# Decay attention, soft MoE and GELU MLP on one core: the logarithm sums computed on the four quarters of the TensorE array

## The chip, the cores and the metric

The kernel runs on one core of a Trainium2 chip. The metric is the device time of one execution in microseconds (us), as the median of several runs.

## The reference

Three stages follow each other. The change touches the first alone: a linear attention with a decay `w` per token and channel (batch 4, 8 heads, 768 tokens, 48 channels a head).

```python
for t in range(S):
    cur = einsum('bhd,bhe->bhde', u * k_t, v_t)
    y_t = einsum('bhd,bhde->bhe', r_t, state + cur)
    state = w_t[..., None] * state + einsum('bhd,bhe->bhde', k_t, v_t)
x = y as (3072 tokens, 384)
logits = x @ phi; slot_in = softmax_over_tokens(logits).T @ x
slot_out[e] = relu(slot_in[e] @ w1[e]) @ w2[e]
x = softmax_over_slots(logits) @ slot_out
h = x @ w_in; out = (h * sigmoid(1.702 * h)) @ w_out
```

## The kernel before

**Tiling.** The attention is done for 16 pairs of heads. In a pair, head 0 has its 48 channels on partitions 0 to 47 and head 1 on 64 to 111 (`HOFF = 64`, `DP = 112`). The 768 tokens are `NC = 6` chunks of 128. Inside a chunk the recurrence is turned into matmuls: `r` is multiplied by the running product of the decays, `k` by its inverse, both counted from the middle token of the chunk (`MID = 64`). The running products come from sums of logarithms:

- ScalarE takes the logarithm of `w` with tokens on partitions (`logs`, L473, into `lw`).
- TensorE sums them (`log_sum`, L897). One matmul a chunk has `lw` (128 tokens by 112 channels) as weights and streams the constant `tri` (128 by 129). `tri` is -1 for the tokens between `t` and the middle in the early half, 1 for those in the late half, and 0 elsewhere: rows 0 to 63 are zero in columns 65 and up, rows 64 to 127 are zero in columns up to 64, and column 64 is all zero. Three chunks lie in bank 0, three in bank 1.
- ScalarE takes the exponentials (`exps`, L498 into `pinv`, L500 into `pw`), 129 columns a chunk.
- VectorE multiplies (`front`, L701 `k` by `pinv`, L703 `r` by `pw`) and forms the decay of a whole chunk, `fdec` (L705).

An fp32 matmul of the source stands as two MATMUL instructions in the trace.

**Order on TensorE in one pair** (`pair`): transposes of `k` (L977), transposes of `x` for the logits (L917, not in every pair), transposes of the pair before's output (L956), state updates (L992), scores (L1010), in every fourth pair the slot logits (L936), the logarithm sums of the *next* pair (L897), the share of the carried state (L1033, which waits for `scaled`), attention times `v` (L1041).

**Order on ScalarE**: copy of the transposed `k` (L506, L508), copies of transposed `x` (L529), `spread_decay` (L515), `logs` of the next pair (L473, which waits for the load `nat` with `w` in it), `scaled_states` (L523, five activations, for L1033), `exps` of the next pair, and the copies of the output (L570).

**Order on VectorE**: scan over the chunk states (L712), the pair before's output into `x_all` (L749, L751, after which a load may reuse that pair's `nat`), masks (L718), `front` of the next pair, bonus (L735, L738, `av_done`).

**Loads.** All loads go through one queue (SP) in a fixed order. In each pair: `rk` of the pair two ahead (L321, 768 KB, waits until L1033 has run), half of an expert's first weights (L336, 768 KB), in every other pair a piece of `w_early` (L341, 192 KB), `v` and `k` with tokens first (L327, 576 KB, waits for `av_done`), `w` and `r` with tokens first (L332, 576 KB, waits for `x_done`, the end of L751). Both halves of `nat` and `rk` have two buffers.

The soft MoE and the MLP that follow are the same in both kernels. In the first pair everything is done in two halves of three chunks (`first_logs`, `first_log_sums`, `first_exps`, `first_front`).

Of the kernel before, what the change touches and what calls it, by code (L numbers as in the profile page):

```python
# [9 lines left out]
ACT = mybir.ActivationFunctionType  # L10
AX = mybir.AxisListType

P = 128
# [3 lines left out]
def decay_attention_soft_moe_gelu_kernel(nc, rk_in, w0_in, nat_in, u_in, phi_in, w1_in, w2_in, win_in, wout_in, out_t):  # L17
# [9 lines left out]
    NC = S // P  # L27
    PPB = u_in.shape[1]
    B = PAIRS // PPB
    HP = 2  # L30
    HD = u_in.shape[2]
    D = HD // HP
    HOFF = 64
    DP = HOFF + D
# [21 lines left out]
    with top:  # L56
# [3 lines left out]
        def sem(name):  # L60
            return top.enter_context(nc.semaphore(name))
# [97 lines left out]
        const_pool = sem("const_pool")  # L159
        const_dve = sem("const_dve")  # L160
        first_ln = sem("first_ln")
        first_logsums = sem("first_logsums")
# [298 lines left out]
        def _(act):  # L461
# [13 lines left out]

            src = [bank[q][0:DP, 0:G3 * (P + 1)].rearrange("p (c t) -> p c t", c=G3) for q in range(2)]

# [9 lines left out]
            def first_exps():  # L487
                for q in range(2):
                    chunks = slice(G3 * q, G3 * (q + 1))
                    act.wait_ge(logsum_done if q else first_logsums, 1)  # L490
                    a.activation(pinv[0:DP, chunks, :], src[q], ACT.Exp, scale=-1.0).then_inc(inv_done, 1)
                    a.activation(pw[0:DP, chunks, :], src[q], ACT.Exp).then_inc(exp_done, 1)

            def exps(s):
                act.wait_ge(f_done, s.i)
                act.wait_ge(logsum_done, s.i + 1)
                for q in range(2):
                    a.activation(pinv[0:DP, G3 * q:G3 * (q + 1), :], src[q], ACT.Exp, scale=-1.0).then_inc(inv_done, 1)  # L498
                for q in range(2):
                    a.activation(pw[0:DP, G3 * q:G3 * (q + 1), :], src[q], ACT.Exp).then_inc(exp_done, 1)  # L500

# [161 lines left out]
        def _(dve):  # L663
# [6 lines left out]
            v.memset(own[:, :, :], 0.0).then_inc(const_dve, 1)  # L670
            v.memset(frep[:, :], 0.0).then_inc(const_dve, 1)
            v.memset(strip[:, :], 0.0).then_inc(const_dve, 1)
            v.memset(old_peaks, -3.0e38).then_inc(peaks_set, 1)
# [9 lines left out]
            def first_front():  # L683

                dve.wait_ge(ld_rk[0], 16)
                r3, k3 = (rk[0][0:DP, z, :].rearrange("p (c t) -> p c t", c=NC) for z in range(2))
# [196 lines left out]
        def _(pe):  # L883
# [11 lines left out]

            def log_sum(c):
                return t.matmul(bank[c // G3][0:DP, (c % G3) * (P + 1):(c % G3 + 1) * (P + 1)], lw[:, c, 0:DP], tri[:, :],  # L897
                                start=True, stop=True)

            def first_log_sums():  # L900
                for c in range(NC):
                    if c % G3 == 0:
                        pe.wait_ge(ln_done if c else first_ln, 1)
                    ins = log_sum(c)
                    if c == G3 - 1:
                        ins.then_inc(first_logsums, 1)
                ins.then_inc(logsum_done, 1)

            def log_sums(s):
                pe.wait_ge(ln_done, s.i + 1)  # L910
                for c in range(NC):
                    ins = log_sum(c)
                ins.then_inc(logsum_done, 1)
# [49 lines left out]
            def pair(s, b=None, xg=None):  # L963
# [7 lines left out]
                for c in range(NC - 1):  # L971
                    if s.first and c == G3:
                        stay_warm(6, 3)
                        pe.wait_ge(exp_done, 2)
                        pe.wait_ge(kc_done, 1)
# [73 lines left out]
            pe.wait_ge(const_pool, 1)  # L1049
            stay_warm(15, 1)  # L1050
            pe.wait_ge(const_pool, 5)
            first_log_sums()
            stay_warm(3, 3)
            pe.wait_ge(const_dve, 4)
# [234 lines left out]
```

## Time and profile before

| | us |
|---|---|
| median of 3 runs | 400.38 (399.33 to 401.03) |
| profiled execution | 400.66 |
| its span, first to last instruction | 398.9 |
| outside the span | 1.8 |
| TensorE busy in the span | 390.8 |
| attention, from the first pair's transposes to the last pair's L1010 and what follows, about | 7.2 to 132.4 |
| soft MoE, about | 132.4 to 176.8 |
| MLP, about | 176.8 to 398.9 |

A group of instructions is called by its line. Times inside the span are counted from its start. TensorE's busy time has matmuls that run side by side counted once.

### The profile page before, as it was taken

The page shows a single profiled execution, that of the slowest core. Times are in us where ns is not written, and L with a number is a line of the kernel's source. Part 1 is how long each engine was busy: PE and PEld are TensorE (multiplying, and loading weights), DVE is VectorE, ACT ScalarE, POOL GpSimd, SP SyncE. Part 2 cuts the span into 40 slices and gives each one's busy share as a digit, 9 for nine tenths or more (in the row PEclk, how much of TensorE's full clock was granted, in tenths as well). Part 3 has the DMA queues.
Part 4 walks back from the last instruction along what each step waited for, and adds up shares of the span by engine and source line. Part 5 has one row for each costly group of instructions (what it writes and reads, how often), then busy time and mean ns, then how long its engine had stood idle before and what let it go on. Part 6 is the DMA issues. An engine that isn't in the chain of part 4 may idle for free.

```text
span 398.9 us, 8722 instructions
## 1 busy us (share of the span) xinstructions
PE 390.8 (98%) x3290; PEld 312.0 (78%) x3290; DVE 242.9 (61%) x453; ACT 187.7 (47%) x418; POOL 49.0 (12%) x50
## 2 busy tenths in 40 slices
PE   7998999999999999999999999999999999999996
PEld 6887888888888743458888888888888888888885
DVE  4888886978788765257765454454545545455451
ACT  4787887878787523065443222422332242223221
POOL 3532442235223200000000000000000000000000
PEclk9999999999999999999999999999999999999999
DMA  8999999999999899930000100200020020002002
GB/s 288 391 359 395 371 362 364 321 354 392 326 364 362 352 424 398 411 163 2 1 2 31 48 2 0 80 0 1 0 79 0 0 79 2 0 2 79 0 2 79
DMA packets 15859, 68.66 MB, mean 172 GB/s; under 512 B 1744, under 2 KB 2896, under 8 KB 14800
## 3 DMA queue, kind: packets, MB, share of 16 engines
q1 hardware_dynamic: 15824, 68.18, 44.5%
q8 instruction: 24, 0.39, 0.4%
q14 instruction: 11, 0.09, 0.1%
HBM read 63.46 MB, written 4.72 MB: 171 GB/s over the span
## 4 chain that ended last, share of the span: by engine, by line
PE 94%; DMA 2%; DVE 1%; issue 1%; ACT 1%; POOL 0%; ACTq 0%; DVEq 0%; SPq 0%; POOLq 0%
PE bank L1231 32%; PE bank L1235 16%; PE bank L1010 6%; PE bank L897 6%; PE bank L1202 6%; PE bank L1041 5%; PE bank L1033 3%; PE bank L1131 3%; PE bank L1151 3%; PE bank L992 2%; PE bank L977 2%; DMA nat<-nat_in 2%; PE bank L956 1%; PE bank L917 1%; PE bank L936 1%; PE bank L894 1%
## 5 line engine op out<-in xcount | busy, mean ns | idle before, releaser
L628 ACT ACTIVATE ring<-bank 128x512 f32<-128x512 f32 x96 | 57.3, 598 | 138.4 <-PE bank L1202 138.3
L866 DVE CAST g_split<-ring 128x512 fp32r<-128x512 f32 x96 | 41.0, 427 | 88.2 <-ACT ring L628 88.2
L1231 PE MATMUL bank<-g_split,wo_hi 128*128 128x512 f32 x285 | 80.1, 389 | 0.0
L1231 PE MATMUL bank<-g_split,wo_lo 128*128 128x512 f32 x285 | 80.0, 389 | 0.0
L1235 PE MATMUL bank<-g_split,wo_hi 128*128 128x512 f32 x285 | 80.0, 389 | 0.0
L868 DVE TENSOR_TENSOR g_split<-ring,g_split 128x512 fp32r<-128x512 f32 x96 | 66.5, 693 | 3.3
L1231 PEld LDWEIGHTS bank<-g_split,wo_lo 128*128 128x128 f32 x285 | 53.5, 188 | 11.1
L1235 PEld LDWEIGHTS bank<-g_split,wo_hi 128*128 128x128 f32 x285 | 53.5, 188 | 11.1
L1231 PEld LDWEIGHTS bank<-g_split,wo_hi 128*128 128x128 f32 x285 | 53.4, 188 | 11.2 <-DVE g_split L866 0.2
L1202 PE MATMUL bank<-cst,mst 128*128 (+1 forms) x96 | 37.4, 391 | 0.0
L446 POOL TENSOR_TENSOR nat<-nat 128x576 f32<-128x576 f32 x16 | 22.6, 1412 | 79.9 <-DMA nat<-nat_in 33.9
L718 DVE TENSOR_TENSOR at<-bank,causal 128x512 f32<-128x512 f32 x48 | 30.0, 681 | 1.5 <-PE bank L1010 1.5
L523 ACT ACTIVATE sc<-tsum,fdec 112x48 f32<-112x48 f32 x80 | 23.5, 369 | 5.1 <-DVE tsum L712 5.1
L1010 PE MATMUL bank<-rk 48*128 48x128 f32 x384 | 25.7, 280 | 0.0
L897 PE MATMUL bank<-tri,lw 128*112 128x129 f32 x192 | 25.7, 284 | 0.0
L897 PEld LDWEIGHTS bank<-tri,lw 128*112 128x112 f32 x192 | 22.4, 180 | 2.6 <-issue 1.1
L1041 PE MATMUL bank<-at,nat 128*48 128x128 f32 x384 | 24.3, 276 | 0.0
L1010 PEld LDWEIGHTS bank<-rk 48*128 48x128 f32 x384 | 22.7, 187 | 1.2 <-issue 0.4
L450 POOL TENSOR_TENSOR nat<-nat,ub 128x576 f32<-128x576 f32 x16 | 22.5, 1409 | 1.3
L1041 PEld LDWEIGHTS bank<-at,nat 128*48 128x48 f32 x384 | 20.2, 123 | 3.0 <-issue 3.0
L701 DVE TENSOR_TENSOR rk<-rk,pinv 112x768 f32<-112x768 f32 x15 | 14.4, 959 | 13.0 <-ACT pinv L498 12.8
L1202 PEld LDWEIGHTS bank<-cst,mst 128*128 128x128 f32 x96 | 17.9, 188 | 3.9 <-ACT mst L623 0.3
(162 smaller groups left out, 424.9 us busy)
## 6 DMA issues: line engine op xcount, KB each, us to landing
nat<-nat_in SPq DMA_DIRECT2D x32, 576.0 KB, 6.5
rk<-rk_in SPq DMA_DIRECT2D x16, 768.0 KB, 6.5
ring<-w_in SPq DMA_DIRECT2D x16, 768.0 KB, 8.1
w2a<-w_in SPq DMA_DIRECT2D x4, 1536.0 KB, 7.4
out_t<-ring SPq DMA_DIRECT2D x5, 768.0 KB, 3.5
ring<-w_in SPq DMA_DIRECT2D x6, 512.0 KB, 6.8
ring<-win_in SPq DMA_DIRECT2D x3, 1024.0 KB, 7.8
ring<-wout_in SPq DMA_DIRECT2D x4, 768.0 KB, 13.4
```

Of the source, the lines that this page charges most:

```text
L446: g.tensor_tensor(rb, rb, kb, ALU.mult).then_inc(bonus_done, 1)
L523: ins = a.activation(sc[0:DP, c, :], tsum[0:DP, :].rearrange("p (e c) -> p e c", e=D)[:, :, c], ACT.Copy, scale=fdec[0:DP, c:c + 1])
L628: a.activation(gact[:, s % NG, :], bank[6 + s % 2][:, :], ACT.Gelu_apprx_sigmoid).then_inc(g_done, 1)
L718: v.tensor_tensor(at[:, 4 * q:4 * q + 4, :], bank[2 + q][:, :].rearrange("p (u t) -> p u t", u=4), causal[:, :].unsqueeze(1).to_broadcast( ...
L866: v.tensor_copy(g_hi[:, s % NG, :], gact[:, s % NG, :]).then_inc(ghi_done, 1)
L868: v.tensor_tensor(g_lo[:, s % NG, :], gact[:, s % NG, :], g_hi[:, s % NG, :].bitcast(F32), ALU.subtract).then_inc(glo_done, 1)
L897: return t.matmul(bank[c // G3][0:DP, (c % G3) * (P + 1):(c % G3 + 1) * (P + 1)], lw[:, c, 0:DP], tri[:, :], start=True, stop=True)
L1010: ins = t.matmul(bank[2 + u // 4][:, P * (u % 4):P * (u % 4 + 1)], k[rows, P * c:P * (c + 1)], r[rows, P * c:P * (c + 1)], start=True, sto ...
L1041: ins = t.matmul(bank[6 + q][half:half + D, P * (c // 2):P * (c // 2 + 1)], nat[s.slot][:, 0, HD * c + D * h:HD * c + D * (h + 1)], at[:, ...
L1202: t.matmul(bank[6 + s % 2][:, :], mst[:, P * f:P * (f + 1)], cst[:, bass.ds((2 * it + n) * TB, TB)], start=True, stop=True).then_inc(h_don ...
L1231: t.matmul(bank[3 * par + o][:, :], wo[:, f, P * o:P * (o + 1)], g_hi[:, s % NG, :], start=(f == 0 and wo is wo_hi), stop=False)
L1235: ins = t.matmul(bank[3 * par + o][:, :], wo_hi[:, f, P * o:P * (o + 1)], g_lo[:, s % NG, :], start=False, stop=(f == FC - 1))
```

## The change

Each logarithm sum is cut into four matmuls, one for each half of the tokens and each head. Each has 64 rows (tokens) and 64 or 48 columns of weights and streams 64 columns of `tri` in place of 129; the zero blocks and the middle column are not computed. The early tokens' sums of all six chunks go to bank 0, the late tokens' to bank 1. The exponentials read a half of the tokens of all six chunks each (six runs of 64 in place of three of 129) and write them into `pinv` and `pw` to the left and right of the middle column. VectorE sets that column to 1 once, at the start. The first pair has its sums in banks 0 and 1, then 2 and 3, and eight exponentials of half the size in place of four. The matmuls that only keep TensorE busy at the start (`stay_warm`, same number) write to bank 4.

```diff
-            src = [bank[q][0:DP, 0:G3 * (P + 1)].rearrange("p (c t) -> p c t", c=G3) for q in range(2)]
+            src = [bank[half][0:DP, 0:NC * MID].rearrange("p (c t) -> p c t", c=NC) for half in range(2)]
+            tokens = [slice((MID + 1) * half, (MID + 1) * half + MID) for half in range(2)]
...
                 for q in range(2):
                     chunks = slice(G3 * q, G3 * (q + 1))
                     act.wait_ge(logsum_done if q else first_logsums, 1)
-                    a.activation(pinv[0:DP, chunks, :], src[q], ACT.Exp, scale=-1.0).then_inc(inv_done, 1)
-                    a.activation(pw[0:DP, chunks, :], src[q], ACT.Exp).then_inc(exp_done, 1)
+                    sums2 = [bank[2 * q + half][0:DP, 0:G3 * MID].rearrange("p (c t) -> p c t", c=G3) for half in range(2)]
+                    for half in range(2):
+                        ins = a.activation(pinv[0:DP, chunks, tokens[half]], sums2[half], ACT.Exp, scale=-1.0)
+                    ins.then_inc(inv_done, 1)
+                    for half in range(2):
+                        ins = a.activation(pw[0:DP, chunks, tokens[half]], sums2[half], ACT.Exp)
+                    ins.then_inc(exp_done, 1)
...
                 for q in range(2):
-                    a.activation(pinv[0:DP, G3 * q:G3 * (q + 1), :], src[q], ACT.Exp, scale=-1.0).then_inc(inv_done, 1)
+                    a.activation(pinv[0:DP, :, tokens[q]], src[q], ACT.Exp, scale=-1.0).then_inc(inv_done, 1)
                 for q in range(2):
-                    a.activation(pw[0:DP, G3 * q:G3 * (q + 1), :], src[q], ACT.Exp).then_inc(exp_done, 1)
+                    a.activation(pw[0:DP, :, tokens[q]], src[q], ACT.Exp).then_inc(exp_done, 1)
...
+            v.memset(pinv[:, :, MID:MID + 1], 1.0).then_inc(mid_set, 1)
+            v.memset(pw[:, :, MID:MID + 1], 1.0).then_inc(mid_set, 1)
...
             def first_front():
+                dve.wait_ge(mid_set, 2)
...
-            def log_sum(c):
-                return t.matmul(bank[c // G3][0:DP, (c % G3) * (P + 1):(c % G3 + 1) * (P + 1)], lw[:, c, 0:DP], tri[:, :],
-                                start=True, stop=True)
+            def log_sum(c, banks, col):
+                for half in range(2):
+                    rows = slice(MID * half, MID * (half + 1))
+                    for h in range(HP):
+                        ch = slice(HOFF * h, HOFF if h == 0 else DP)
+                        ins = t.matmul(bank[banks[half]][ch, MID * col:MID * (col + 1)], lw[rows, c, ch],
+                                       tri[rows, (MID + 1) * half:(MID + 1) * half + MID], start=True, stop=True)
+                return ins
...
-                    ins = log_sum(c)
+                    ins = log_sum(c, (2 * (c // G3), 2 * (c // G3) + 1), c % G3)
...
-                    ins = log_sum(c)
+                    ins = log_sum(c, (0, 1), c)
...
-                        stay_warm(6, 3)
+                        stay_warm(6, 4)
...
-            stay_warm(15, 1)
+            stay_warm(15, 4)
             pe.wait_ge(const_pool, 5)
             first_log_sums()
-            stay_warm(3, 3)
+            stay_warm(3, 4)
```

## Rows read from the trace of the kernel before

**Rows 1.** The page: busy time, and the granted clock in 40 slices.
```profile
PE 390.8 (98%) x3290; PEld 312.0 (78%) x3290; DVE 242.9 (61%) x453; ACT 187.7 (47%) x418; POOL 49.0 (12%) x50
PEclk9999999999999999999999999999999999999999
```

**Rows 2.** Busy time by stretch: us, each engine (x instructions), clock, DMA share, GB/s.
```profile
7.22:37.72 30.50, 28.62 (x444) 25.08 (x445) 24.26 (x43) 22.62 (x60) 11.27 (x8) 1.00 1.00 386
...
70.44:102.88 32.44, 32.16 (x485) 27.96 (x484) 26.63 (x48) 25.84 (x68) 11.29 (x8) 1.00 0.96 354
102.88:132.40 29.52, 29.30 (x440) 25.46 (x438) 24.95 (x46) 22.87 (x62) 11.27 (x8) 1.00 0.93 341
```

**Rows 3.** Timeline of TensorE in one pair: start, us, line, names, shapes, count.
```profile
85.49 0.70 PE L977 MATMUL bank<-ident,rk 112*128 112x112 f32 x5
...
87.64 0.66 PE L992 MATMUL bank<-nat,kcn 128*48 128x48 f32 x20 [0.22 <-issue]
88.22 1.61 PE L1010 MATMUL bank<-rk 48*128 48x128 f32 x24
89.76 1.57 PE L897 MATMUL bank<-tri,lw 128*112 128x129 f32 x12
...
92.05 1.52 PE L1041 MATMUL bank<-at,nat 128*48 128x128 f32 x24
```

**Rows 4.** The same timeline: L1033 in four pairs that follow each other.
```profile
91.26 0.86 PE L1033 MATMUL bank<-rk,sc 48*48 48x128 f32 x20
...
100.42 0.86 PE L1033 MATMUL bank<-rk,sc 48*48 48x128 f32 x20
...
107.96 0.86 PE L1033 MATMUL bank<-rk,sc 48*48 48x128 f32 x20
...
115.69 0.86 PE L1033 MATMUL bank<-rk,sc 48*48 48x128 f32 x20
```

**Rows 5.** Windows of 0.11 us: L1033 alone at its start, then L897 alone.
```profile
91.26:91.37 0.11, 0.11 (x4) 0.11 (x8) 1.00 0.49 182
...
89.75:89.86 0.11, 0.10 (x1) 0.10 (x2) 1.00 1.33 559
```

**Rows 6.** Timeline of ScalarE in the same pair, and two later logarithms.
```profile
88.98 0.68 ACT L473 ACTIVATE lw<-nat 128x576 f32<-128x576 f32 x1 [0.95 <-DMA nat<-nat_in]
89.57 1.46 ACT L523 ACTIVATE sc<-tsum,fdec 112x48 f32<-112x48 f32 x5
91.37 0.88 ACT L498 ACTIVATE pinv<-bank 112x387 f32<-112x387 f32 x2 [0.33 <-PE bank L897]
...
96.61 0.68 ACT L473 ACTIVATE lw<-nat 128x576 f32<-128x576 f32 x1 [0.57 <-DMA nat<-nat_in]
...
112.56 0.69 ACT L473 ACTIVATE lw<-nat 128x576 f32<-128x576 f32 x1
```

**Rows 7.** ScalarE's waits for the loads, 0 to 190 us: total us, times, longest.
```profile
ACT lw L473 <- DMA nat<-nat_in: 7.5, 9, 2.0
```

**Rows 8.** Timeline of the load queue: `rk` three times, and one load of `w` and `r`.
```profile
84.30 0.33 SPq L321 DMA_DIRECT2D rk<-rk_in  x1
...
89.92 0.34 SPq L332 DMA_DIRECT2D nat<-nat_in  x1
92.31 0.33 SPq L321 DMA_DIRECT2D rk<-rk_in  x1
...
101.47 0.33 SPq L321 DMA_DIRECT2D rk<-rk_in  x1
```

**Rows 9.** The chain that ended last, 18 to 40 us: start, us, what.
```profile
21.14 0.96 DVE rk L701
...
23.82 0.77 DVE nat L738
...
24.80 6.95 DMA nat<-nat_in
```

**Rows 10.** ScalarE's first logarithm from a load of `nat`.
```profile
10.46 0.68 ACT L473 ACTIVATE lw<-nat 128x576 f32<-128x576 f32 x1 [0.83 <-DMA nat<-nat_in]
```

More of the change, by code:

```diff
@@ L160, in decay_attention_soft_moe_gelu_kernel @@
         const_dve = sem("const_dve")
+        mid_set = sem("mid_set")
         first_ln = sem("first_ln")
```

## The prediction

> **What bounds the kernel now.** I read the page first. TensorE is busy for 390.8 of 398.9 us, and its clock is granted in full throughout [rows 1]. So a saving has to come out of TensorE's own stream, unless another engine or a load is close behind. The division by stretches shows that in the attention the loads are close behind: from 7.2 us to 132.4 us the DMA engines are busy 93 to 100% of the time at 341 to 386 GB/s [rows 2]. The change touches nothing after the attention, so only these 125 us can move.
>
> The timeline of one ordinary pair shows how tight TensorE's stream is: the next group starts when the last one ends, with one gap of 0.22 us, and L1033 starts 1.50 us after L897 [rows 3, 4]. L1033 repeats after 9.16, 7.54 and 7.73 us; the long step is the one with the slot logits in it [rows 4]. A batch of four pairs takes 32.44 us [rows 2].
>
> The second stream is ScalarE's. Its logarithm (L473) stood 0.95 us idle for the load of `w`, then came five activations (L523) that end at 91.03, and TensorE's L1033, which needs them, starts at 91.26 [rows 4, 6]. So behind TensorE's stream lies a chain from a load that is late by only about 0.2 us. It waited for a load nine times, 7.5 us in all [rows 7].
>
> **The change, part by part.**
>
> *The sums.* Now: 12 matmuls of 129 columns, 1.50 us from L897's start to L1033's [rows 3, 4]. They run one at a time: in 0.11 us at the group's start one is in flight. In the same length of time L1033 has four in flight, which are its two heads by two places in the output [rows 5]. The new sums have that form: two halves of rows by two halves of columns, so I take them four wide. They are 6 chunks x 4 quarters x 2 = 48 instructions, 12 rounds of four. The length of a round follows from three groups, each taken as rounds plus a fixed change-over c: L1010 has 24 matmuls, two wide, of 128 columns, 12 rounds in 1.54 us; L1033 has 5 rounds of 128 columns in 0.79 us; so 7 rounds are 0.75 us, a round of 128 columns is 0.107 us and c = 0.25 us. L992 has 10 rounds of 48 columns (two wide) in 0.58 us, so 0.033 us a round with the same c [rows 3, 4]. For 64 columns that gives 0.033 + 16 x 0.074/80 = 0.048 us, and 12 x 0.048 + 0.25 = 0.83 us. The weights of a quarter are wider than L992's (64 against 48), which can hold a round up: at 0.060 us the sum is 0.97. I take 0.85. TensorE gives back 1.50 - 0.85 = 0.65 us a pair, 0.55 to 0.75. There are 15 such groups (16 pairs less the first, whose sums come before the pairs): 9.8 us if all of it stayed.
>
> The Trainium skill (TensorEngine Tiling (Array Packing), Key Properties) says that a change of tiling mode drains the engine. The mean change-over of 0.25 us that I find agrees that a change of shape costs something. By the page the new sums and L1033 would be of one mode, and one of the two drains around the sums would go as well; the gain would lie at the upper end, 0.75 us, where I take 0.65.
>
> *The exponentials.* Four activations of 384 in place of 387 elements, in other runs: nothing. VectorE still waits for both `pinv`, so no product starts earlier or later than the sums allow.
>
> *The first pair.* Half as wide activations, eight in place of four, on ScalarE; shorter sums on TensorE. Whatever it gives is cut off at 10.46 us, when ScalarE takes its first logarithm from `nat` after 0.83 us of waiting for that load [rows 10]; its issue does not depend on the sums. I count 0. It costs something only if it loses more than that 0.83 us.
>
> *The column of ones.* Two memsets on VectorE before the first data; its first product waits for ScalarE and loads. Nothing.
>
> **What is late next.** With TensorE 0.65 us faster, L1033 would start at 90.61 in the pair shown, but its operands are there at 91.03 + 0.1 [rows 6]. The chain goes round over two pairs:
> - L1033 starts, and 1.05 us later `rk` of the pair two ahead is issued (91.26 to 92.31) [rows 4, 8];
> - from that issue until the logarithm can use the last load of the same pair: 84.30 to 96.61, 12.3 us; at a place where the queue ran emptier 101.47 to 112.56, 11.1 us. I take 11.7 [rows 6, 8];
> - L473 to L523 0.59, L523 1.46, wake-up 0.1: 2.15 us [rows 6]; then L1033 starts.
>
> Sum: 1.05 + 11.7 + 2.15 = 14.9 us for two pairs (14.3 to 15.5). TensorE alone would need, from L1033 to L1033: 7.73 - 0.65 = 7.08 in an ordinary pair, 9.16 - 0.65 = 8.5 with the slot logits, and 7.54 less about 0.1 of waiting less 0.65 = 6.8 after it [rows 4]. Two steps beside each other make 7.08 + 7.08 = 14.2, 15.6, 15.3 and 6.8 + 7.08 = 13.9. Where that is under 14.9 the loads set the time. In the steady state the second step after the slot logits stretches from 7.1 to 8.1 us (14.9 - 6.8), and the others stay: 6.8 + 8.1 + 7.1 + 8.5 = 30.5 us a batch. That is 1.9 us under 32.44, not 2.6. At 15.5 us for the loads it is 31.1 (1.3 less than now), at 14.3 it is 29.9 (2.5 less).
>
> So: batch from 37.7 to 70.4 and batch from 70.4 to 102.9, -1.9 to -2.2 each, together -4.1 (the first is the longer one by 0.3). In the last stretch three sums remain, and its loads ran emptier: -1.4.
>
> *The first four pairs* (7.2 to 37.7) have DMA at 100% [rows 2]. Their chain goes from L701 at 21.14 over L738 (23.82) to a load of `nat` that takes 6.95 us, and TensorE waits for it [rows 9]. The exponentials ahead of L701 come earlier by what two groups of sums give back, less what scaled states hold up: the first by about 0.2 (the load at 10.46 holds), the second by about 0.65, 0.9 to 1.1 in all. What the third and fourth save is lost behind the load. -1.0.
>
> Sum: -1.0 - 4.1 - 1.4 = -6.5 us. The profiled execution has 400.66 us, 398.9 of span and 1.8 outside, 0.3 over the median. 400.66 - 6.5 = 394.2; against the median 400.4 - 6.5 = 393.9. I say 394.0.
>
> **After the attention.** The expert weights are loaded behind the last pairs' events. They move with them, and no wait of TensorE for them is in my sum; if the loads of the attention end less early than TensorE does, up to 1 us can be lost there.
>
> **The rivals.**
> - *Nearly all of the gain stays* (12%). Earlier issues close the pauses of the queue, the round over the loads drops below 14 us, and 15 x 0.65 to 0.75, less 1 at the start, is 9 to 10: 390.5 to 391.5. For it: 386 GB/s were moved in the first stretch against 354 later [rows 2]. Against it: the load of 6.95 us lies just there [rows 9].
> - *The loads take all* (14%). The DMA engines are busy 93 to 100% [rows 2]; if the time of a pair's loads from first issue to last use grows from 11.7 to about 12.7 us as they come closer together, the round is 15.9 us, a batch of two rounds 31.8 us, and the stretches give 0.6 to 0.9 each: with the start 3 us or less, 397.5 to 400.
> - *The quarters run two wide* (5%). Then 24 rounds of 0.048 and 0.25 make 1.40 us against 1.50: 1.5 us at most, 399 to 400.5. Against it is L1033 [rows 5].
> - *Slower: the quarters run one after another* (5%). 48 matmuls each by itself, at 0.048 us, with the change-over make 2.55 us: +1.05 a pair, 15 times, 416. It turns slower from (1.50 - 0.25)/48 = 0.026 us a matmul on; four wide I have 0.012. Against it are the four in flight in L1033; for it, that L1033 shows them at 128 columns only.
> - The Trainium skill (TensorE: Matmul & The Clock Gate, Back-to-back issue gap) has a limit by number: with hardware decode off the sequencer spends about 62 ns on each MATMUL. As a mechanism here it is the same rival at another price, 1.3 us a pair and more. L992 issues 20 matmuls in 0.58 us, 29 ns each [rows 3], so the trace is against it and I give it 1% of its own: the 48 would take at least 48 x 0.029 = 1.39 us if 29 ns were a limit of issue, which is no change (399), and at the page's figure 2.98 us, which would give 422.
>
> **How the numbers follow.** The case of the sum has 60%, with 391.5 to 396.5 of its own. The others hold 12, 14, 5, 5 and 1; 3 are for what I don't see. The range is 390.5 to 399.0: it takes in the full gain and most of the case in which loads take all. A difference under 0.5%, 2.0 us, is about what this measurement can't tell from none. Faster by more: 60 + 12 + a third of 14 + 1 = 78%. Within 0.5%: the rest of the loads' case, two wide, and some of the unseen, 16%. Slower: 6%.
>
> **What the profile after would show.** L897's group with 48 matmuls a pair, and the start of L1033 0.8 to 0.9 us after its start where nothing is waited for. Right for the middle of the sum: L1033 or L473 waits for the load in ordinary pairs, ScalarE's wait for L897 (0.33 us in the pair shown [rows 6]) is gone in these, and its wait for `nat` stands; batches of 30 to 31 us; GB/s up to 375 or so. Wrong if a pair's L897 takes over 1.2 us (the width or the round is mistaken), if batches take 29.3 us (the loads gave way), or if TensorE stands for L992's load in every pair. The MLP must take the same time as before.

## The result and the profile after

The changed kernel takes 407.88 us (407.81 to 408.09, 4 runs) beside 400.70 us for the kernel before on the same chip (399.33 to 401.07, 4 runs). The ratio is 1.0186, with a 95% interval of 1.0161 to 1.0212: slower by 7.2 us. A few executions of a kernel fall in a slower state with a lower granted clock (the slowest took 539 us at 0.66): medians in this document are of all runs, ratios leave those runs out. I had forecast 394.0, and 399.0 as the upper end. The profiled execution has a span of 406.4 us against 398.9.

In the changed kernel the lines of TensorE are numbered anew: L897 is L911 (the sums), L956 L971, L977 L992, L992 L1007, L1010 L1025, L1033 L1048, L1041 L1056.

The page after, its lines on busy time, clock, DMA and queues:

```profile
PE 385.2 (95%) x3866; PEld 305.2 (75%) x3866; DVE 243.3 (60%) x455; ACT 187.8 (46%) x422; POOL 49.1 (12%) x50
...
PE   7979998798899999999999999999999999999996
...
PEclk9988999999999999999999999999999999999999
DMA  8997999799799799980000200200020010002001
GB/s 296 400 367 256 362 400 362 245 359 384 260 344 377 307 404 396 418 352 2 2 0 0 80 0 2 78 0 1 0 77 0 0 59 19 2 0 77 2 1 77
...
q8 instruction: 28, 0.46, 0.4%
```

TensorE is busy for 5.6 us less than before [rows 1], and the kernel is 7.5 us longer: TensorE stands. The DMA engines fall to 245 to 260 GB/s in three slices. The instruction queue has 28 packets of 16 KB where the page of before has 24; with 256 instructions to a packet that is 64 bytes each. TensorE has 7,732 weight loads and matmuls against 6,580, and 231 other instructions (semaphores and registers) in both.

The attention by stretches of four pairs each, as in [rows 2]:

```profile
6.71:41.50 34.79, 29.99 (x589) 25.68 (x589) 24.41 (x43) 22.67 (x61) 11.29 (x8) 0.90 0.93 348
41.50:75.60 34.10, 30.03 (x629) 25.81 (x628) 26.18 (x45) 25.70 (x68) 11.32 (x8) 1.00 0.91 342
75.60:109.77 34.17, 29.81 (x629) 25.60 (x627) 27.36 (x49) 25.77 (x68) 11.30 (x8) 1.00 0.93 337
109.77:138.60 28.83, 26.50 (x535) 22.68 (x533) 23.31 (x42) 22.76 (x61) 11.13 (x8) 1.00 0.91 336
```

The first stretch lasts 34.79 us, where it had 30.50 [rows 2]; the second and third are longer by 1.4 and 1.7, the last is 0.7 shorter. That is 6.7 us more of attention. It starts 0.5 us earlier, and the soft MoE behind it takes 1.3 us more (138.6 to 184.3 against 132.4 to 176.8), which makes the 7.5. The same loads now flow at 336 to 348 GB/s. The MLP has its 222.1 us in both.

The sums themselves did what I had worked out. One pair on TensorE's timeline:

```profile
36.78 1.61 PE L1025 MATMUL bank<-rk 48*128 48x128 f32 x24
38.31 0.92 PE L911 MATMUL bank<-tri,lw 64*64 64x64 f32 x48
39.26 0.86 PE L1048 MATMUL bank<-rk,sc 48*48 48x128 f32 x20
```

L1048 starts 0.95 us after L911 (0.94 in most other pairs where nothing is waited for, 0.86 in the first), where it was 1.50 [rows 3, 4]. Now the pair before this one:

```profile
27.27 0.28 PE L1025 MATMUL bank<-rk 48*128 48x128 f32 x2
27.48 0.92 PE L911 MATMUL bank<-tri,lw 64*64 64x64 f32 x48
28.42 0.44 PE L1048 MATMUL bank<-rk,sc 48*48 48x128 f32 x8
31.28 0.65 PE L1048 MATMUL bank<-rk,sc 48*48 48x128 f32 x12 [2.42 <-issue]
31.86 2.80 PE L1056 MATMUL bank<-at,nat 128*48 128x128 f32 x24
```

After 8 of the 20 matmuls of L1048 TensorE does nothing for 2.42 us, and goes on with the ninth. All 20 lie behind one and the same wait for `scaled`, so no semaphore can hold the ninth; the trace finds no releaser ("issue"). Then the granted clock has fallen, and the next group lasts 2.80 us in place of 1.52. What else stood still, by windows of 1 us:

```profile
27.50:28.50 1.00, 0.98 (x54) 0.87 (x56) 1.00 (x2) 0.78 (x3) 0.82 (x1) 1.00 0.89 358
28.50:29.50 1.00, 0.35 (x8) 0.16 (x9) 0.77 (x2) 0.97 (x3) 0.00 (x0) 1.00 1.01 181
29.50:30.50 1.00, 0.00 (x0) 0.00 (x0) 0.99 (x2) 0.67 (x2) 0.00 (x0) 1.00 0.84 281
30.50:31.50 1.00, 0.22 (x9) 0.22 (x10) 1.00 (x3) 0.00 (x0) 0.00 (x0) 1.00 0.50 203
31.50:32.50 1.00, 1.00 (x18) 0.80 (x12) 0.90 (x2) 0.00 (x0) 0.00 (x0) 0.64 0.12 39
32.50:33.50 1.00, 1.00 (x14) 0.98 (x12) 0.44 (x1) 0.08 (x1) 0.48 (x1) 0.50 0.41 74
```

The clock is at 1.00 (2.4 GHz) until TensorE has stood idle, then at 0.50 (1.2 GHz). That happened after two of the seven stops counted below, and not after the others:

```profile
21.55:24.96 3.41, 3.41 (x23) 3.02 (x23) 1.36 (x2) 1.47 (x4) 0.56 (x1) 0.50 1.01 409
31.79:35.20 3.41, 3.41 (x30) 2.95 (x28) 1.05 (x2) 0.98 (x2) 1.40 (x1) 0.50 0.59 206
71.30:76.00 4.70, 2.99 (x56) 2.62 (x56) 1.70 (x2) 2.51 (x6) 0.00 (x0) 1.00 0.43 134
105.42:110.00 4.58, 2.69 (x49) 2.32 (x50) 1.93 (x4) 2.46 (x6) 0.00 (x0) 1.00 0.47 131
```

The first two rows follow stops of 1.52 and 2.42 us. The last two begin with stops of 1.71 and 1.89 us, and the clock stays at 1.00. The DMA engines run dry, down to 39 GB/s, because the next load of `rk` waits for L1048. The load queue's own timeline shows that:

```profile
23.68 0.34 SPq L328 DMA_DIRECT2D nat<-nat_in  x1
27.64 0.34 SPq L333 DMA_DIRECT2D nat<-nat_in  x1
32.10 0.33 SPq L322 DMA_DIRECT2D rk<-rk_in  x1
32.65 1.03 SPq L337 DMA_DIRECT2D ring<-w_in  x1
```

No load is issued from 27.64 to 32.10. So this stop costs three times: 2.4 us of TensorE, 1.3 us of half clock in the next group, and a hole in the loads, on which the pairs after it live. At the stops from 71 and 105 us the clock held, and the DMA engines were busy for only 43% and 47% of these stretches.

TensorE's waits of this kind from 7 to 135 us, among matmuls:

```profile
PE bank L1048 <- issue: 4.3, 2, 2.4
PE bank L1056 <- issue: 3.1, 2, 1.6
...
PE bank L911 <- issue: 1.7, 1, 1.7
...
PE bank L992 <- issue: 1.0, 1, 1.0
PE bank L932 <- issue: 0.8, 1, 0.8
```

They sum to 10.9 us. In the kernel before the same sum is 0.8.

**Where the stops lie.** I counted all of TensorE's records (weight loads, matmuls, semaphore and register instructions) from the start of the trace to each stop, and took from the packed trace the start of the instruction queue's packet ahead of it. (With weight loads and matmuls alone there is no common remainder.)

```
stop (us)        at          count  mod 256  packet starts  TensorE goes on after
 20.03 -> 21.55  in L1056      705     193       19.00            2.55
 28.86 -> 31.28  in L1048      961     193       28.74            2.54
 63.03 -> 64.62  in L1056     2241     193       62.29            2.33
 71.30 -> 73.01  in L911      2497     193       70.54            2.47
 98.18 -> 99.18  in L992      3521     193       96.69            2.49
105.42 -> 107.31 ahead L1048  3777     193      104.96            2.35
132.97 -> 133.77 in L932      4801     193      131.45            2.32
```

All of them leave 193 on division by 256, and 256 instructions are one packet of 16 KB. TensorE goes on some 2.4 us after the packet's start. So it stands where it needs the next block of its own instructions and that block hasn't come.

The record says more when every crossing (a count that leaves 193) is set beside its packet, not only those with a stop. From 7 to 135 us the changed kernel has 18 crossings with a packet ahead of each, one packet to one crossing. Seven are the stops above, and one more is a wait of 0.1 us. TensorE passes the other ten without waiting, and there the packet had started 3.4 us or more before. Over all thirteen kernels of this document there are 205 such crossings. At each of the 26 with a wait of over 0.2 us, TensorE goes on 2.2 to 2.6 us after the packet's start. At the 174 without any wait the packet had started 2.5 us or more before. The packets themselves take 0.9 to 1.1 us in the changed kernel and 0.9 to 1.7 in the one before, so the transfer isn't what grows: what is late is its start. In the changed kernel a packet starts 1.0 to 7.2 us after the crossing before it. Where that was 4.2 us or more TensorE stopped; where it was 3.7 or less it waited for 0.1 us at most.

The kernel before has nearly the same delays (up to 4.3 us) and no stop. Its crossings are 8.5 us apart in the mean, and 4.3 + 2.6 = 6.9 us fit in; the changed kernel's are 6.9 us apart with its stops, and 6.2 us in the run without the expert loads below. The Trainium skill (Runtime: NRT & Kernel Launch, Instruction fetch mechanics) says that an engine's instructions come in blocks of 256 over a DMA queue of its own, the next while the current one is used, and that the cost of a crossing is "mostly hidden". The packets and the places of the stops agree with the first part. That it is hidden holds for the kernel before, and not here: TensorE's waits are 0.8 to 2.4 us at seven of 18 crossings.

An ordinary pair before (one with transposes of `x`, without slot logits) has 238 instructions of TensorE, all kinds counted, the same pair after 310: 12 matmuls of the sums became 48, each with its weight load. The packets are 0.4% of the DMA engines' time, so it isn't their bytes; it is when they arrive, on engines that are 91 to 93% busy with loads.

### The profile page after: what moved, and what is told of

It reads as the page before. It is cut to its first block, busy times and chain, and to the rows that moved or that the text cites. A ratio compares the mean times of both kernels' runs of the same rounds, so it can differ in the third digit from the quotient of the medians.

```text
span 406.4 us, 9881 instructions
## 1 busy us (share of the span) xinstructions
PE 385.2 (95%) x3866; PEld 305.2 (75%) x3866; DVE 243.3 (60%) x455; ACT 187.8 (46%) x422; POOL 49.1 (12%) x50
## 4 chain that ended last, share of the span: by engine, by line
PE 84%; DMA 6%; issue 4%; DVE 2%; ACT 2%; DVEq 0%; SPq 0%; ACTq 0%
PE bank L1246 32%; PE bank L1250 16%; PE bank L1217 5%; PE bank L1056 5%; DMA nat<-nat_in 5%; PE bank L1025 3%; PE bank L1146 3%; PE bank L1166 3%; PE bank L1048 3%; PE bank L992 2%; PE bank L911 2%; PE bank L1007 2%; PE bank L951 1%; PE bank L971 1%; ACT sc L530 1%
## 5 line engine op out<-in xcount | busy, mean ns | idle before, releaser
L1056 PE MATMUL bank<-at,nat 128*48 128x128 f32 x384 | 26.9, 291 | 3.1 <-issue 3.1
L1056 PEld LDWEIGHTS bank<-at,nat 128*48 128x48 f32 x384 | 22.2, 130 | 6.4 <-issue 6.2
L1025 PE MATMUL bank<-rk 48*128 48x128 f32 x384 | 25.7, 280 | 0.0
L1025 PEld LDWEIGHTS bank<-rk 48*128 48x128 f32 x384 | 22.7, 187 | 1.2 <-issue 0.4
L577 ACT ACTIVATE yts<-bank 112x384 f32<-112x384 f32 x32 | 15.8, 492 | 15.6 <-PE bank L1056 14.6
L1048 PE MATMUL bank<-rk,sc 48*48 48x128 f32 x320 | 14.0, 276 | 7.6 <-issue 4.3
L722 DVE TENSOR_TENSOR_SCAN tsum<-frep,bank 112x240 f32<-112x240 f32 x16 | 10.4, 653 | 17.7 <-PE bank L1007 10.5
```

The lines of the kernel that those rows point to most:

```text
L1025: ins = t.matmul(bank[2 + u // 4][:, P * (u % 4):P * (u % 4 + 1)], k[rows, P * c:P * (c + 1)], r[rows, P * c:P * (c + 1)], start=True, sto ...
L1048: ins = t.matmul(bank[6 + c % 2][half:half + D, P * (c // 2):P * (c // 2 + 1)], sc[rows, c - 1, :], r[rows, P * c:P * (c + 1)], start=(c < ...
L1056: ins = t.matmul(bank[6 + q][half:half + D, P * (c // 2):P * (c // 2 + 1)], nat[s.slot][:, 0, HD * c + D * h:HD * c + D * (h + 1)], at[:, ...
```

## The experiments

The theory of the trace: the number of instructions, together with full DMA engines, makes TensorE outrun its instruction stream. The rivals: the shorter sums bring the loads into each other's way; the 48 small matmuls or the two-bank layout of the sums cost something in themselves; more busy time on TensorE is what costs. Each time is a median; each ratio is to runs of the kernel before on the same chip, whose medians were 400.8 to 401.7 us.

### The loads of expert weights taken out of the attention

In both kernels the half-expert loads into `ring` (768 KB a pair) and the pieces of `w_early` are issued behind the attention's last load, all at once:

```diff
-                    load_w1(m, q)
-                    if q == 1:
-                        load_w2_early(m - 1)
...
             sp.wait_ge(x_done, 2 * PAIRS - 2)
+            for e in range(NE):
+                for q in range(2):
+                    load_w1(e, q)
+                load_w2_early(e)
```

> The kernel before, with the 16 half loads of the experts' first weights and the 8 pieces of w_early issued only after the attention (12.6 + 1.6 MB of 45 MB leave the attention; the result is complete, and the soft MoE must wait for them, so the total is longer). It is the base of the next run. All theories: the attention no longer waits for loads, so it comes near TensorE's own sum of groups, 7.2 us for a pair without and 7.7 with transposes of x: its last L1010 group starts 3 to 5 us earlier than 129.65 us. No stop of TensorE inside a group over 0.3 us.

> The changed kernel with the same loads moved behind the attention. Theory A (TensorE stops because its instruction stream, fetched in blocks of 16 KB, 256 instructions, by the same DMA engines, waits behind the queued loads): with a third of the loads gone the fetches arrive in time, no stop at a multiple of 256 instructions is over 0.3 us, and the attention ends 7 to 10 us before that of the run above; the total is shorter by the same 7 to 10 us. Theory B (the four-quarter form itself disturbs the groups after it, L1033's and L1041's forms): the stops inside the groups stay, 8 us and more in all. Theory C (the loads of data are late, TensorE waits for them): the stops go too, as in A.

Measured: 428.62 us (428.13 to 429.37) with the old sums, 422.26 (421.50 to 423.35) with the new. The new ones are 6.4 us faster. The weights now come late for the soft MoE, in both; the attention is what can be compared. The last group of the scores (L1010 in the kernel before) starts at 128.09 in the one and at 121.69 in the other, 6.4 us earlier. I had expected 7 to 10. The old sums alone gained 1.6 us of attention by the loads' absence (129.65 in the kernel before), where I had expected 3 to 5. Old sums, then new sums, over the attention:

```profile
7.00:128.00 121.00, 119.21 (x1810) 103.77 (x1808) 100.71 (x177) 95.81 (x253) 43.75 (x31) 1.00 0.76 253
```

```profile
7.00:121.50 114.50, 109.65 (x2348) 95.06 (x2348) 100.57 (x176) 95.06 (x253) 43.73 (x31) 1.00 0.79 268
```

The second kernel issues all the instructions of the changed kernel (19 packets in the attention, as there), and has not one matmul waiting for "issue" from 7 to 135 us. With DMA engines 79% busy the stream arrives in time: the packets start at most 3.5 us after the crossing before, and at no crossing does TensorE wait. The quarters, their layout and the exponentials together are worth 6.4 us here, so no cost of theirs can explain the loss. What takes that away, and 7.2 us more, needs the full DMA engines.

### Instructions alone, in the kernel before

36 matmuls of one column with their weight loads are put ahead of each pair's sums; the sums stay as before. That is the changed kernel's number of instructions, 310 a pair. The control has a single matmul of 120 columns.

```diff
             def log_sums(s):
                 pe.wait_ge(ln_done, s.i + 1)
+                for n in range(36):
+                    c0 = NS * (n % 4)
+                    t.matmul(bank[0][c0:c0 + NS, BANK - 4:BANK - 3], ones_b[:, 0:NS], ones_b[:, 0:1], start=True, stop=True)
```

> The kernel before, with 36 tiny bf16 matmuls (128 rows, 32 columns of weights, 1 column streamed) ahead of the logarithm sums of each pair, written to unused columns of bank 0: 72 more instructions a pair on TensorE, as in the changed kernel, and no quarters. They cost TensorE 0.5 to 0.7 us a pair themselves (15 times, 7 to 10 us). Theory A: besides that, stops of 0.3 to 2.5 us, 256 instructions apart, also inside groups, at places where no semaphore is waited for; fewer than after the change, since a pair is longer; 409 to 418 us. Theories B and C: no stop inside a group; 405 to 410 us.

> The control of the run above: one bf16 matmul of 128 rows, 128 columns of weights and 120 columns streamed in the same place, 2 more instructions a pair. It costs 0.1 to 0.3 us a pair. All theories: no stop inside a group, 401 to 404 us. It says what a pure addition of TensorE time does to the total (whether 15 x its cost appears in full).

Measured: 409.58 us (408.35 to 409.99), ratio 1.0218 (1.0183 to 1.0253), and 401.34 (400.33 to 403.34), ratio 0.9997 (0.9974 to 1.0021). The first shows how a stop looks with nothing of the change in the kernel:

```profile
44.32 0.82 PE L897 MATMUL bank<-tri,lw 128*112 128x129 f32 x6
45.08 0.42 PE L1036 MATMUL bank<-rk,sc 48*48 48x128 f32 x2
46.90 0.81 PE L1036 MATMUL bank<-rk,sc 48*48 48x128 f32 x18 [1.41 <-issue]
```

This stop is at count 1473, the others at 961, 1217 and 4033: 193 again, four times. Waits for "issue" are 3.5 us, 3.3 of them at these four. The time lies in the range that I gave the theory, but at 409.58 it is also inside the rival's 405 to 410, and only the stops decide. And the control didn't match: the 36 matmuls delay the sums by 0.33 us a pair, the one of 120 columns by 0.07. Of the 8 us, about 15 x 0.33 = 5 may be work. A better control followed.

```diff
+                for _ in range(5):
+                    t.matmul(bank[0][:, 3 * (P + 1):3 * (P + 1) + 120], ones_b[:, 0:P], ones_b[:, 0:120], start=True, stop=True)
```

> The kernel before with 5 matmuls of 120 columns ahead of each pair's sums: by the row of the run with one such matmul (the next group starts 0.07 us after it) about 0.35 us of TensorE a pair, the 0.33 us of the 36 tiny ones, but 10 instructions a pair in place of 72 (248 in place of 310). Theory (the count decides): under 1.5 us of 'issue' waits in 7 to 135 us, no stop over 0.5 us at a recorded count that leaves 193 on division by 256, and at most the added work, 15 x 0.35 = 5.2 us, so 401.5 to 406.5. Rival (busy time on TensorE is what costs, whatever its instructions): the 409.6 of the run with 36 tiny ones, 408 or more.

Measured: 403.29 us (402.16 to 405.18, 12 runs), ratio 1.0059 (1.0041 to 1.0077), with 0.4 us of "issue" waits and no stop at a crossing. The five matmuls delay the sums by 0.28 us a pair (92.16 to 92.44), a little less than the 36 with 0.33: 15 x 0.05 = 0.8 us in all. With that work, 248 instructions a pair cost 2.5 us, and 310 cost 8. The rest, between 4 and 5 us, is what the number of instructions costs (an estimate from these medians), and the stops (3.3 us) are the part of it that the trace shows directly.

### The number of instructions between 226 and 310

The sums on halves of the tokens, with both heads in one matmul (262 instructions a pair):

```diff
-                    for h in range(HP):
-                        ch = slice(HOFF * h, HOFF if h == 0 else DP)
-                        ins = t.matmul(bank[banks[half]][ch, MID * col:MID * (col + 1)], lw[rows, c, ch],
-                                       tri[rows, (MID + 1) * half:(MID + 1) * half + MID], start=True, stop=True)
+                    ins = t.matmul(bank[banks[half]][0:DP, MID * col:MID * (col + 1)], lw[rows, c, 0:DP],
+                                   tri[rows, (MID + 1) * half:(MID + 1) * half + MID], start=True, stop=True)
```

and a mixture, chunks 0 to 2 on halves and 3 to 5 on quarters (286):

```diff
-                    for h in range(HP):
-                        ch = slice(HOFF * h, HOFF if h == 0 else DP)
+                    for h in range(HP) if c >= G3 else range(1):
+                        ch = slice(HOFF * h, HOFF if h == 0 else DP) if c >= G3 else slice(0, DP)
```

> The changed kernel with only two matmuls a chunk, one for each half of the tokens with all 112 channels (64 rows, 112 columns of weights, 64 streamed): 24 fewer MATMULs and as many LDWEIGHTS a pair than the change, 262 instructions a pair. The weights take longer to load than 64 columns to stream, so I expect 1.1 to 1.4 us from the group's start to L1033's. Theory A: fewer and shorter stops than after the change, 0 to 4 us in all; 398 to 404 us, under the change. Theory B (the form of 64 by 64 disturbs): no stops.

> Three chunks in halves, three in quarters, 286 instructions a pair: the middle of the dose. Theory A: between the run above and the change, 400 to 407 us, with stops at multiples of 256 instructions of 2 to 8 us in all. Theory B: stops in proportion to the quarters, anywhere.

The kernel before's layout with one-pass fp32: the logarithms and a copy of the constant are of the type F32R, so each sum is one matmul in place of two, of 130 columns (226 instructions a pair, shorter sums; how exact they still are was not measured). A second kernel adds the 36 tiny matmuls to it (298):

```diff
-        lw = sb(gen1, "lw", [P, NC, P])
+        lw = sb(gen1, "lw", [P, NC, P], F32R)
...
-                return t.matmul(..., lw[:, c, 0:DP], tri[:, :], ...)
+                return t.matmul(..., lw[:, c, 0:DP], trir[:, :], ...)
```

> The kernel before, loads untouched, with the logarithms and the triangle stored as fp32r, so that a sum is one instruction of MATMUL and one of LDWEIGHTS in place of two each (130 columns, 128 rows, 112 columns of weights; the sums are less exact). L897's group should take 0.7 to 1.0 us, as the four quarters did, but with 12 instructions a pair in place of 96 (24 before). Theory A (the instruction stream): the gain stays, no stop at a block of 256 instructions, 393 to 397 us. Theory C (the loads of data take whatever TensorE gives back, or make it worse): 399 us or more.

> The same with the 36 tiny matmuls of the earlier run, 72 more instructions and 0.33 us a pair. TensorE's sum is then about that of the changed kernel plus 0.2 us a pair, with 298 instructions a pair (310 after the change, 238 before, 226 in the run above). Theory A: stops of 0.3 to 2.5 us come back at multiples of 256 instructions; 402 to 410 us. Theory C or a plain sum: the run above + 5 us, 398 to 402 us, no such stops.

Measured, with the "issue" waits of matmuls from 7 to 135 us and the part of them at crossings:

| kernel | instructions a pair | us | ratio to before | issue waits | at crossings |
|---|---|---|---|---|---|
| one pass | 226 | 399.46 | 0.9972 (0.9930 to 1.0014) | 1.3 | 0 |
| before | 238 | 400.70 | | 0.8 | 0 |
| before, 5 more | 248 | 403.29 | 1.0059 (1.0041 to 1.0077) | 0.4 | 0 |
| halves | 262 | 399.83 | 0.9978 (0.9946 to 1.0010) | 2.7 | 0 |
| mixture | 286 | 404.99 | 1.0093 (1.0054 to 1.0133) | 6.0 | 5.4 |
| one pass, 36 more | 298 | 406.41 | 1.0118 (1.0078 to 1.0159) | 6.7 | 5.8 |
| before, 36 more | 310 | 409.58 | 1.0218 (1.0183 to 1.0253) | 3.5 | 3.3 |
| quarters | 310 | 407.88 | 1.0186 (1.0161 to 1.0212) | 10.9 | 10.9 |

One of these runs went against me. I had expected 393 to 397 us of the one-pass kernel, and 399 or more by the rival that the loads take back what TensorE gives. It has no stop at a crossing and took 399.46 us, which can't be told from the kernel before: the rival came true there. So two things stand side by side, the loads that take back the gain and the stops that turn it into a loss.

The profiled execution of the halves took 405.94 us, 6 more than their median, so its row of waits counts for little. The mixture is faster on its sums than the halves (1.04 against 1.24 us a pair) and 5 us slower as a whole. Its four stops of 0.9 to 1.9 us are at 1473, 1729, 1985 and 3777, five of the one-pass kernel with 36 more (0.3 to 2.3 us) at 1473, 1729, 3009, 3265 and 3521. These are 193 again, one and all. By time alone the one-pass pair says less: 36 more cost 6.9 us, of which 15 x 0.33 = 5 may be work. The longest:

```profile
50.69 0.81 PE L902 MATMUL bank<-trir,lw 128*112 128x130 f32 x6
51.43 0.74 PE L1041 MATMUL bank<-rk,sc 48*48 48x128 f32 x17
54.52 0.66 PE L1041 MATMUL bank<-rk,sc 48*48 48x128 f32 x3 [2.34 <-issue]
```

The last three of a group of 20 wait 2.34 us. Between 262 and 286 instructions a pair, a time that can't be told from the kernel before turns into a loss. The sum of "issue" waits is that of one execution each, and does not by itself order the kernels.

### The same work, the blocks moved by half

The changed kernel, with 128 more instructions once, ahead of everything, while TensorE waits for the first logarithms:

```diff
             stay_warm(15, 4)
+            for n in range(64):
+                c0 = NS * (n % 4)
+                t.matmul(bank[4][c0:c0 + NS, BANK - 4:BANK - 3], ones_b[:, 0:NS], ones_b[:, 0:1], start=True, stop=True)
```

> The changed kernel with 64 tiny matmuls (128 TensorE instructions, half a block of 256) issued once at the start, while TensorE waits for the first logarithms anyway. Nothing of the pairs is touched. Theory (TensorE stands still where its instruction stream crosses into a block that the full DMA engines haven't brought yet): the stops without a semaphore still come at recorded counts that leave 193 on division by 256, so about 128 instructions earlier in the work than in the changed kernel, not at the same lines (before: L1056 at 20.03, L1048 at 28.86, L911 at 71.08 and 105.20, L992 at 97.87, L932 at 132.70); the sum of TensorE's 'issue' waits in 7 to 135 us lies between 6 and 14 us (10.9 in the changed kernel), the time between 404 and 411 us. Rival (the stops belong to the work: to certain groups, banks or operands that the quarters leave behind): they stay at the same lines and times, shifted by under 0.7 us, whatever the count. Second rival (single events of one execution, unrelated to either): other places with no common remainder.

Measured: 409.31 us (406.05 to 411.73), ratio 1.0166 (1.0106 to 1.0227), as slow as the changed kernel. The two longest stops:

```profile
52.75 0.39 PE L1048 MATMUL bank<-rk,sc 48*48 48x128 f32 x3
54.99 0.70 PE L1048 MATMUL bank<-rk,sc 48*48 48x128 f32 x17 [1.85 <-issue]
...
87.62 0.44 PE L1048 MATMUL bank<-rk,sc 48*48 48x128 f32 x8
90.13 1.09 PE L1048 MATMUL bank<-rk,sc 48*48 48x128 f32 x12 [2.07 <-issue]
```

Every stop of 0.9 us or more that no semaphore explains is at a new place in the work and at the same remainder: 1729, 1985, 3265, 4289, 4545, all 193. The places in the work where the changed kernel stopped are passed without one. So the stops belong to the blocks of the stream and not to a group, a bank or an operand. "Issue" waits are 8.7 us.

### The gain without the instructions

The halves in one-pass fp32: 12 matmuls of 64 columns a pair, 238 instructions, as many as before.

```diff
-                    for h in range(HP):
-                        ch = slice(HOFF * h, HOFF if h == 0 else DP)
-                        ins = t.matmul(bank[banks[half]][ch, MID * col:MID * (col + 1)], lw[rows, c, ch],
-                                       tri[rows, (MID + 1) * half:(MID + 1) * half + MID], start=True, stop=True)
+                    ins = t.matmul(bank[banks[half]][0:DP, MID * col:MID * (col + 1)], lw[rows, c, 0:DP],
+                                   trir[rows, (MID + 1) * half:(MID + 1) * half + MID], start=True, stop=True)
```

> The sums on two halves of the tokens, both heads in one matmul, with the logarithms and the constant in the one-pass fp32 type: 12 matmuls of one pass for each pair in place of 48, some 238 TensorE instructions a pair, the number of the kernel before. Theory (the number of instructions a pair decides whether the stream arrives in time, the shorter sums are a real gain of 0.7 to 1.2 us on a pair, most of which the loads take back): under 1.5 us of 'issue' waits in 7 to 135 us, and 395 to 399.5 us, faster than the kernel before by 0.5 to 1.6 %. Rival (what made the changed kernel slow is the two-bank layout of the sums and the exponentials that go with it, which this kernel shares): 404 us or more.

Measured: 397.93 us (395.88 to 405.31, 10 runs), ratio 0.9914 (0.9876 to 0.9953): faster than both kernels, by 2.9 us than the one before. At no crossing does TensorE wait. Its "issue" waits are 1.9 us, where I had expected under 1.5; all of them are ahead of L1009, and none is at a crossing. It has the layout of the quarters, so the layout isn't what costs. Where nothing is waited for, L1050 (the share of the state) starts 0.70 us after the sums:

```profile
65.43 0.78 PE L913 MATMUL bank<-trir,lw 64*112 64x64 f32 x12
66.13 0.86 PE L1050 MATMUL bank<-rk,sc 48*48 48x128 f32 x20
...
87.93 0.78 PE L913 MATMUL bank<-trir,lw 64*112 64x64 f32 x12
89.38 0.86 PE L1050 MATMUL bank<-rk,sc 48*48 48x128 f32 x20 [0.68 <-ACT sc L532]
```

In the second pair it stands 0.68 us for the scaled states. Over all pairs, from 7 to 135 us:

```profile
ACT lw L476 <- DMA nat<-nat_in: 12.2, 15, 2.2
PE bank L1050 <- ACT sc L532: 8.4, 13, 1.0
...
PE bank L1009 <- issue: 1.9, 3, 0.9
```

Thirteen times TensorE waits for the states and 15 times ScalarE for the load of `w` (nine times, 7.5 us, before [rows 7]). That is the chain that I had worked out.

## Why the prediction was wrong

The step that failed is the one in which I counted the sums' edit by its duration alone: "TensorE gives back 1.50 - 0.85 = 0.65 us a pair", with the 48 instructions as 12 rounds of four. The rounds were right. What was left out is that 36 more matmuls and 36 more weight loads a pair have to be fetched, over DMA engines that [rows 2] shows 93 to 100% busy. I took these as a limit for the loads only. The runs showed in its place that TensorE waits 10.9 us at the crossings of its instruction blocks, where my sum had nothing. My rivals on the number of instructions asked how fast TensorE can issue them, not whether they have arrived.

- *The size of the sums*: 0.94 or 0.95 us in nearly every pair without a wait, forecast 0.85, range to 0.97. The form was right, and the saving is 0.55 us a pair (1.50 less 0.95), the low end of my 0.55 to 0.75. Over 15 groups that is 8.2 us and not 9.8. The rivals "two wide" and "one after another" fell. So did the rival by the 62 ns a matmul that I took from the Trainium skill (TensorE: Matmul & The Clock Gate, Back-to-back issue gap), and its other price of 29 ns: 48 in 0.92 us are 19 ns each.
- *The exponentials, the first pair, the ones*: the kernels without the expert loads differ by 6.4 us in all, and the halves in one pass have the layout and are faster. No cost of theirs is to be seen beside that.
- *What is late next*: I let the round over the loads set the time after the sums. In the changed kernel it didn't: L1048 waited for the scaled states 3.0 us in all, and for "issue" 4.3. In the halves with one pass, where the stream holds, it did, 8.4 us. Its size was off there: from the start of every fourth L994 to the next (36.61, 68.59, 100.20) a batch takes 32.0 and 31.6 us, and I had 30.5, with 31.8 in the rival "the loads take all". That rival gave 397.5 to 400, and the measured 397.93 lies in it. The sums of that kernel are shorter than the quarters', so this bears on the mechanism and not on the very number. The one-pass sums without the quarters' layout took 399.46, also without a stop at a crossing. So the second term that was off is the round over the loads: even with the stream in time, no kernel here came to 394.0.
- *The first four pairs*: forecast -1.0, measured +4.3. Two stops lie there (20.0 and 28.9, 3.9 us), and the attention's only two stretches at half clock.
- *The batches*: forecast -1.9 to -2.2 each, measured +1.4 and +1.7. *The last stretch*: -1.4, measured -0.7.
- *After the attention*: up to 1 us could be lost there, I said; 1.3 us are lost in the soft MoE. The MLP is unchanged, as forecast.
- *Slower*: I gave it 6% in all, with 5 for matmuls one after another. That case's mechanism did not occur; the sign came true by something that no case of mine held.

The account: relative to quarters with free DMA engines (-6.4) the changed kernel loses 13.6 us. The stops are 10.9 of these; the kernel before has none at a crossing. The clock was at 0.50 for 2 x 3.41 us (21.55 to 24.96 and 31.79 to 35.20), which is up to 3.4 us more. That the stops, the clock and the loads' holes add up is worked out, not shown: the stops and the clock alone make 14.3, so they overlap, and the loads would have taken part of the gain in any case, as the halves with one pass show.

What stays open: when a block's fetch is asked for, and what it then waits for. The trace has no record of the request. The packets' starts say this much: a packet starts at most 1.1 us ahead of the crossing before it, and mostly after. So each block comes while the one before it is used, and hardly earlier. Their mean delay after that crossing is 3.3 us in the changed kernel and 1.9 us in the same kernel without the expert loads (3.0 and 1.3 us with the old sums). That fits a packet that waits among the loads on its DMA engine, and doesn't show it. That a less busy DMA removes the stops was shown.

## What to carry to other kernels

Count instructions as well as time when a matmul is cut into smaller ones that run side by side: a shorter group is no gain if the stream that feeds the engine is fetched over DMA engines that are full. Read the room from two numbers of the trace: the time in which the engine uses up 256 instructions, and how long after a crossing the next packet starts, with 2.6 us on top. Here a kernel with 8.5 us against 6.9 at most had no stop, and one with 6.9 us against up to 9.8 (7.2 and 2.6) had seven. A stop inside a group, without a semaphore, at a constant remainder modulo 256 of the count of all the engine's instructions, is the mark of it, and moving the blocks with idle instructions is a cheap test. Shorten with fewer instructions first: here 12 matmuls of one pass on half the tokens won 0.9%, in a type whose exactness has to be measured before it is used, where 48 on quarters lost 1.9%.

## What the runs showed of the hardware

- TensorE stood 0.8 to 2.4 us at seven of 18 crossings of 256 instructions with DMA engines 91 to 93% busy, at 310 instructions a pair, and it stood at crossings in every kernel with 286 or more under the full loads; with DMA engines 79% busy it did not, at 310.
- At each of 26 crossings with a wait of over 0.2 us TensorE went on 2.2 to 2.6 us after the start of the block's packet of 16 KB, in five kernels alike, though the packet itself took about 1.0 us.
- A stop of 2.42 us was followed by a granted clock of 0.50: 24 matmuls took 2.80 us in place of 1.52. Stops of 1.59, 1.71 and 1.89 us in the same run were not: the clock stayed at 1.00.
- 48 matmuls of 64 x 64 x 64 columns, as four quarters, took 0.92 us, 19 ns each. 12 one-pass matmuls of 64 columns, of 64 rows by 112, took 0.78.
- A matmul of 120 columns of bf16 put ahead of a group delayed the group by only 0.07 us, though its record says 0.23; five of them delayed it by 0.28.
